# Where the softmax, the splits of x and the token sums stand around the end of the attention stage of a fused attention and two-layer MoE kernel

## What is computed

```
out_up    = repeat(softmax_attention(mean of 4 positions of q, k, v), 4)    # 144 x 144 per head
out_local = softmax_attention(q, k, v, only where |i - j| < 4)
x  = (out_up + out_local) as [2304, 512]
xn = x / sqrt(mean(x * x over 512) + 1e-6) * rms_g
y  = (silu(xn @ w_gate) * (xn @ w_val)) @ w_out                             # 512 -> 1536 -> 512
r  = maximum(y @ w_in, 0);  out = (r * r) @ w_out2                          # 512 -> 2048 -> 512
```

## Time and profile before

| | us |
|---|---|
| timed executions | 944.83, 945.67, 957.65; median 945.67 |
| profiled execution, its own time | 942.91 |
| its span | 941.1 |
| mean granted clock of TensorE | 0.992 of full |
| TensorE busy | 916.4 (97%) |
| DVE, ScalarE, GpSimd busy | 644.5, 447.3, 595.9 |

### The profile page before, as it was taken

The page is one execution under the profiler, slowest core; times in us unless marked ns, Lnnn a source line. Parts: engine busy times, 40 slices in busy tenths (PEclk is TensorE's granted clock), DMA queues, the critical chain, the costliest instruction groups (busy, mean ns, idle before and its releaser), DMA issues.

```text
span 941.1 us, 17729 instructions
## 1 busy us (share of the span) xinstructions
PE 916.4 (97%) x6056; PEld 829.9 (88%) x6056; DVE 644.5 (68%) x964; ACT 447.3 (48%) x1147; POOL 595.9 (63%) x627
## 2 busy tenths in 40 slices
PE   7999989999999999999999999999999999999998
PEld 6777778999989999989999988898989898989896
DVE  7999956789885778875555796667864466744443
ACT  4788965444565444465444465242533233423221
POOL 3688778787888778877777764556564445544420
PEclk9998989999999999999999999999999999999999
DMA  9965012222111111111111221212030101030101
GB/s 256 261 172 165 21 57 79 69 68 68 46 46 46 45 47 46 45 46 46 46 45 46 91 68 46 90 45 68 23 112 24 46 23 46 23 112 23 46 1 67
DMA packets 57673, 63.94 MB, mean 68 GB/s; under 512 B 5616, under 2 KB 50544, under 8 KB 57200
## 3 DMA queue, kind: packets, MB, share of 16 engines
q1 hardware_dynamic: 56000, 61.63, 22.3%
q10 hardware_dynamic: 1584, 1.18, 0.4%
HBM read 58.07 MB, written 4.72 MB: 67 GB/s over the span
## 4 chain that ended last, share of the span: by engine, by line
PE 78%; DVE 3%; issue 1%; ACT 1%; POOL 0%; DMA 0%; ACTq 0%; DVEq 0%
PE bank L1460 43%; PE bank L1515 21%; PE bank L1490 14%; DVE xs L1100 1%; DVE prod L1173 0%; ACT xs L753 0%; DVE vt L1167 0%; ACT wst L717 0%; PE bank L1470 0%; POOL wst L595 0%; DVE wst L1107 0%; DMA out_dram<-xT 0%; DVE gt L1167 0%; DVE wo L1212 0%; ACT xT L836 0%
## 5 line engine op out<-in xcount | busy, mean ns | idle before, releaser
L1460 PE MATMUL bank<-xs,wst 128*128 128x384 f32 x2520 | 503.2, 339 | 4.8 <-DVE vt L1167 2.1
L1460 PEld LDWEIGHTS bank<-xs,wst 128*128 128x128 f32 x2520 | 441.0, 188 | 28.9 <-issue 7.5
L595 POOL TENSOR_TENSOR wst<-wraw,wst 128x256 fp32r<-128x256 f32 x240 | 233.6, 991 | 126.1 <-ACT wst L717 124.4
L1515 PE MATMUL bank<-wo,gs 128*128 128x512 f32 x864 | 218.4, 393 | 1.4 <-ACT xT L836 0.8
L1490 PE MATMUL bank<-hb,wo 128*128 128x512 f32 x864 | 189.0, 336 | 1.3 <-DVE hb L1185 1.3
L1515 PEld LDWEIGHTS bank<-wo,gs 128*128 128x128 f32 x864 | 160.4, 188 | 29.8 <-DVE gs L1206 1.1
L1490 PEld LDWEIGHTS bank<-hb,wo 128*128 128x128 f32 x864 | 146.0, 188 | 9.9 <-issue 1.6
L1167 DVE TENSOR_TENSOR vt<-u,bank 128x384 f32<-128x384 f32 x120 | 66.2, 552 | 123.8 <-PE bank L1460 123.7
L717 ACT CAST wst<-wraw 128x256 fp32r<-128x256 f32 x360 | 123.4, 406 | 4.9 <-DMA wraw<-w_dram 2.7
L578 POOL TENSOR_TENSOR wraw<-wraw,stage 128x256 f32<-128x256 f32 x60 | 50.1, 835 | 105.9 <-DMA wraw<-w_dram 105.7
L797 ACT ACTIVATE sig<-gt 128x384 f32<-128x384 f32 x72 | 37.8, 526 | 121.4 <-DVE gt L1167 120.3
(11 more groups left out here) (110 smaller groups left out, 1034.2 us busy)
## 6 DMA issues: line engine op xcount, KB each, us to landing
wraw<-w_dram SPq DMA_DIRECT2D x180, 128.0 KB, 2.3
stage<-w_dram SPq DMA_DIRECT2D x60, 128.0 KB, 2.2
woraw<-w_dram SPq DMA_DIRECT2D x28, 256.0 KB, 3.0
vquad<-v_dram SPq DMA_DIRECT2D x16, 288.0 KB
out_dram<-xT SPq DMA_DIRECT2D x18, 256.0 KB, 3.0
vwin<-v_dram SPq DMA_DIRECT2D x28, 140.0 KB
kp<-k_dram SPq DMA_DIRECT2D x3, 1152.0 KB, 9.8
qs<-q_dram SPq DMA_DIRECT2D x3, 1152.0 KB, 15.3
```

The costliest lines, as they stand in the source:

```text
L595: nc.gpsimd.tensor_tensor(b[:, 1, :], w_source(w, p), b[:, 0, :].bitcast(fp32), ALU.subtract).then_inc(wlp_done, 1)
L1460: last = mm(XY[s % 2][:, 0:HC], wst[:, u % 2, p, pw, 128 * k:128 * k + 128], xs[:, p, px, k, :], start=(p not in CONTINUES and i == 0 and ...
L1515: last = mm(ACC[t][:, :], gs[:, v % 2, m, px, 128 * t:128 * t + 128], wo[:, 2 * j + m, pw, :], start=(j == 0 and n < 18 and i == 0), stop= ...
```

## The change

- The six token sums leave unit 37 and stand in pairs in units 36, 37 and 38. The 12 root steps of DVE start in unit 39 instead of 38.
- Attention's loop: ScalarE casts parts 0 and 1 of x in units 49 and 50; before, all seven stood in units 48 to 51. DVE subtracts part 0 in unit 50 only; before, parts 0 to 3 in units 49 to 51. GpSimd's two combinations of x go from units 49 and 50 to 48 and 51.
- Tail: ScalarE's other five casts and DVE's subtractions 1 to 4 stand between the attention's last steps, with the sums of unit 51 before most of them. GpSimd normalises unit 51 before its first subtraction of x. TensorE makes each group of unit 0's products one attention unit later.

```
-SUMS_AT = 37
-ROOT_AT = (38, 38, 39, 39, 39, 39, 40, 40, 40, 40, 41, 41)
+SUMS_AT = (36, 36, 37, 37, 38, 38)
+ROOT_AT = (39, 39, 39, 39, 40, 40, 40, 40, 41, 41, 41, 41)
...
-COMBINE_X_AT = (48, 49, 49, 50)
-X_HIGH_AT = (48, 49, 49, 50, 50, 51, 51)
-X_LOW_AT = (49, 50, 50, 51)
+COMBINE_X_AT = (48, 49, 48, 51)
+X_HIGH_AT = (49, 50)
+X_LOW_AT = (50,)
...
 # GpSimd, tail
+            normalise(G_ALL - 1)
             x_low(5)
-            normalise(G_ALL - 1)
             x_low(6)
...
 # ScalarE, tail
             keep_output(G_ALL - 6)
             take_turned(G_ALL - 4)
-            first_copy(0)
+            x_high(0, 2)
             keep_output(G_ALL - 5)
             take_turned(G_ALL - 3)
+            x_high(0, 3)
+            first_copy(0)
             keep_output(G_ALL - 4)
-            copy_11(0)
+            x_high(0, 4)
             take_turned(G_ALL - 2)
             keep_output(G_ALL - 3)
+            x_high(0, 5)
+            copy_11(0)
             take_turned(G_ALL - 1)
+            x_high(0, 6)
+            keep_output(G_ALL - 2)
             sigmoid(0, 0)
-            keep_output(G_ALL - 2)
             keep_output(G_ALL - 1)
...
 # DVE, tail
+            x_low(0, 1)
+            sums(G_ALL - 1)
+            x_low(0, 2)
+            x_low(0, 3)
             x_low(0, 4)
             add(0, 1)
-            sums(G_ALL - 1)
             for p in range(3, NP):
                 add(0, p)
...
 # TensorE
-            def token_sums():
-                pe.wait_ge(ss_add, 3)
-                pe.wait_ge(exp_done, FOUR_BANKS)
-                for t in range(TT):
-                    last = mm(SS[:, t:t + 1], ssq[:, 128 * t:128 * t + 128], ones[:, 0:1], start=True, stop=True,
-                              skip_group_check=True)
-                last.then_inc(ss_mm, 1)
+            def token_sums(t):
+                if t == 0:
+                    pe.wait_ge(ss_add, 3)
+                    pe.wait_ge(exp_done, FOUR_BANKS)
+                last = mm(SS[:, t:t + 1], ssq[:, 128 * t:128 * t + 128], ones[:, 0:1], start=True, stop=True,
+                          skip_group_check=True)
+                if t == TT - 1:
+                    last.then_inc(ss_mm, 1)
...
-                if g == SUMS_AT:
-                    token_sums()
+                for t in range(TT):
+                    if SUMS_AT[t] == g:
+                        token_sums(t)
...
             transposes(G_ALL - 4)
             values(G_ALL - 5)
-            product(0, 0)
             transposes(G_ALL - 3)
             values(G_ALL - 4)
+            product(0, 0)
+            transposes(G_ALL - 2)
+            values(G_ALL - 3)
             product(0, 1)
             product(0, 2)
-            transposes(G_ALL - 2)
-            values(G_ALL - 3)
+            transposes(G_ALL - 1)
+            values(G_ALL - 2)
             product(0, 3)
             product(0, 4)
-            transposes(G_ALL - 1)
-            values(G_ALL - 2)
+            values(G_ALL - 1)
             product(0, 5)
             product(0, 6)
-            values(G_ALL - 1)
```

More of the change, by code:

```diff
@@ L773, in _ @@
                     squares(0, SQUARES_AT.index(g))
-                for p in range(NP):
+                for p in range(len(X_HIGH_AT)):
                     if X_HIGH_AT[p] == g:
```

## The result

The changed kernel is slower, by little: a median of 956.55 us (12 executions, 946.21 to 960.32) against 946.23 for the kernel before in the same session (12 executions, one of them of 5052.8 us, which no mean below has in it); ratio 1.0075, 95% interval 1.0049 to 1.0102. A second session gave 955.45 against 949.89, ratio 1.0041 (1.0005 to 1.0076). The means from here on leave out the six executions that lay over 1.5% above the fastest of their kernel and count as slow. Over its two sessions the changed kernel's mean is 954.4 us (23 executions, 955.2 and 953.6); the kernel before has 948.0 in the first session (11 executions) and 949.2 to 950.0 in four later ones of 29 to 35. The forecast was 944.9, 0.8 us faster, in 940.8 to 949.5.

What follows compares the result with a forecast made beforehand. TensorE, busy 97%, was taken as the bound up to product (2,1), with GpSimd's chain binding after (0,3). Terms 0.25 + 1.5 + 1.5 - 2.5 = 0.75, say 0.8 us off the 945.67 median, gave 944.9 us, range 940.8 to 949.5.

Steps and rivals of the forecast that it cites:

- Part 1: Token sums spread over units 36 to 38: slow stretch there goes, 1.5 us gained, bounds 0 and 2.8.
- moved: Rival: grown wait at the second spread lowers the clock near 106 us; 1.9 us won, 943.8; chance 0.15.
- the likeliest case: Whole kernel: the parts sum to about 0.8 us won, median 944.9 us; chance 0.35.
- I take it that the clock stays up: Spread-out sums, units 36 to 38: full clock is kept, worth 2.8 us on TensorE, at most 3.4.
- Part 2: ScalarE's order, units 48 to 51: fewer casts, so transpose 48's second half starts at 121.1 instead of 122.55 us.
- DVE's work up to there is unchanged: Up to the maxima for unit 49's exponent (115.22 us): unit 48's removed cast brings nothing at first.
- Part 3: Softmax's tail up to product (0,3): 1.5 us won at full clock, 2.5 us lost to half clock.
- 1.5 us are won at full clock: Tail: product (0,3) ends at 131.8 us instead of 133.3.
- Half clock follows again: After the tail's waits, values 47 to about product (0,1) run at half clock, costing 2.5 us.
- Part 4: Product (0,3) to (2,1): GpSimd's chain bounds it, 15.5 us, shortened by only 0.25; TensorE's gain is lost waiting.
- The slower rival: New slow stretch in unit 2 after waits ahead of (2,0) and (2,1): 2.6 us slower, 948.2; chance 0.25.

Runs made afterwards that it cites:

- e1: Kernel before with only the change's token sums and root steps: 953.9 us mean, ratio 1.0051.
- before_again: Second profile of the kernel before, unchanged: 949.98 us.
- e8: Kernel before with only the change's token sums and root steps, and the second spread in unit 47 instead of 46: 950.1 us mean, ratio 0.9987.
- e11: As e10, but GpSimd's combination of x back in unit 49 instead of 48: 945.2 us mean, ratio 0.9941.
- e10: Changed kernel with token sums over 64 columns and unread matmuls filling waits at the second spread, values 46, transposes 48 and 49: 947.8 us mean, ratio 0.9986.
- e7: Changed kernel with unread matmuls filling waits at the second spread, values 46, transposes 48 and 49; one-column sums: 950.5 us mean, ratio 0.9995.
- e9: Kernel before with token sums over 64 columns and unread matmuls at the second spread, values 46 and transposes 48: 947.1 us mean, ratio 0.9969.
- e14: The kernel of e9 timed once more: 945.4 us mean, ratio 0.9959 against the kernel before.
- after_again: Changed kernel once more, unchanged, for a second profile: 953.6 us mean, ratio 1.0041 against the kernel before.
- e4: Kernel before with only the second spread one unit earlier, 45 in place of 46: 954.1 us mean, ratio 1.0037.
- after: First session and profile of the changed kernel: median 956.55 us, ratio 1.0075 against the kernel before.
- e2: The change without its token sums and root steps, which stay as in the kernel before: 952.3 us mean, ratio 1.0026.

## Why the prediction was wrong

**Part 1.** "That is the gain of part 1: 1.5 us." The size of the wait was right: 1.92 us in place of 0.92, where I had 2.2. What failed is its price. The forecast's own sum has it as the part of the gain that doesn't get through, with no clock in it; only the rival "moved" (this very wait) lowers the clock there, with a chance of 0.15. And that rival prices it as a gain on the forecast: 1.5 us late at units 48 to 51, against 2.5 us saved later. (Its sum should read 0.75 - 1.5 + 2.5 = 1.75 us won, not 1.9.) I priced slow stretches by the two in my trace, 6.7 us each. In three profiles with a wait of 1.9 us (both of the changed kernel, and e1) the stretch lasted 27 to 31 us, over all the attention that was left. At half clock the small matmuls of the attention held TensorE busy nearly throughout, so the waits of the earlier trace rows vanished, and the work took up to twice as long. From the second spread to product (2,1) it is 47.0 us in e1, whose tail is the old one, against 41.8 in before_again: 5.2 us lost where the rival had 1.0 won. In the changed kernel it is 8.6 us. The place was right, and half clock after the wait too; its length and so its price were wrong, and the likeliest case left it out.

The gain itself isn't there either. "I take it that the clock stays up" held in the changed kernel's profiles and e1's and failed in six others; in the mean the spread-out sums are worth nothing (e8), because a slow stretch began at sums of one column in six of nine profiles with three units of them, and in four of five with one. At sums of 64 columns it did in none of four.

**Part 2.** "DVE's work up to there is unchanged" was the second failing step. It was unchanged in its list, but not in its neighbour: I had GpSimd's combination in my account as work and didn't check what it would meet. With the combination moved back (e11), ScalarE's copies of transposes 46 and 47 stand 7.6 and 10.4 us behind the start of qk 48, as my 117.60 and 120.45 less 110.0 have them, and product (0,3)'s load is issued 21.9 us behind it (137.02 - 115.12), where my sum at full clock has the product's end at 131.8 - 110.0 = 21.8. In e10 and e7 the load is at 23.1, so the collision cost 1.2 us. The prediction quoted the rule for it, the shared port pair of the Trainium skill (SBUF — State Buffer, SBUF: two separate sides), and used it on the chain behind (0,3) only. The trace agrees with the rule: both instructions have two SBUF inputs, and the later one came out longer by about what it had to wait (1.2 us longer, 1.35 from its start to the end of GpSimd's).

**Part 3.** In the changed kernel's profile, which is at half clock there, the sums of unit 51 can't be judged; in e11 they come 12.5 us behind the start of qk 48, where I had 12.7. "1.5 us are won at full clock" set a new tail at full clock against an old one that was partly slow. The old order at full clock has that load at 22.5 us (e9, e14), so the new one wins 0.6 at like clock, with the collision taken out. "Half clock follows again" held for the unfilled waits: at the softmax's end every profile without fills in the tail has slow time, 7 to 14 us of it, unless the long stretch already covers it.

**Part 4** held in most profiles, though not in the one shown first. From the load behind product (0,3) to product (2,1) it is 15.3 us in the kernel before (133.57 to 148.86). With the new tail it is 14.8 to 15.0 in eight profiles of ten, after_again among them: 0.3 to 0.5 shorter, where I expected 0.25. TensorE's wait on GpSimd there is then 0.6 us as before, and the rest of its idle time lies ahead of it (0.74 and 0.89 us on DVE in after_again). In the changed kernel's first profile and in e10 it is 15.5: GpSimd's four additions take 6.2 to 6.3 us instead of 5.5, two of the four 1.9 to 2.0 us long instead of one, and TensorE waits 1.8 us, where I expected about 2. In either case what TensorE won was lost there, as said.

**The slower rival** (a slow stretch in unit 2, chance 0.25) named the right sign at the wrong place, which is luck and not insight: no profile has a slow stretch there, after waits of 0.66 and 1.84 us among dense products. The Trainium skill's warning on short idles between groups of matmuls (TensorE: Matmul & The Clock Gate, A second HAM failure mode: psum-queue depth-cycling) fits the attention, where the wait at the spread shows it (full clock up to 114.8 us and half from 114.9 in the changed kernel, full throughout in e10 with the wait filled), and not the products.

**The base.** One profile and three times were too few for a kernel whose executions spread over 13 us. The forecast of 944.9 lies 3 to 5 us below the means of the kernel before (948.0 to 950.0). That isn't what put the result outside the range: in its own session the kernel before had a median of 946.23, 0.6 above the 945.67 that I took, and the changed one 956.55. With the base 4.3 us higher the range would end at 953.8, still under both medians of the changed kernel.

## What to carry to other kernels

Take a part of work off TensorE's path and it arrives earlier at its next wait; where it works in small matmuls, that wait can cost several times its length, by the clock (here 1 us more of waiting, 5 us lost in e1's profile). Look at what it arrives at, and if nothing useful fits, fill the wait with matmuls nobody reads, or give thin ones more columns where that costs next to nothing. And when a GpSimd instruction is moved, look at DVE's list in its new place, not only at its own queue.

## What was not expected of the hardware

- A stretch at half clock had no one length in the attention: 3 us (e4 after the spread, before_again at the sums), 10 us (e8) and 29 us or more (after) were seen, with TensorE busy all through. What ends one within the attention stays open. The three long ones ended among unit 0's products.
- An idle of 0.9 to 4.9 us in which TensorE waits for nothing that the profile shows, near 20, 30 or 55 us, is in every profile, and slow stretches of 3 to 21 us begin near it in all but the first profile of the kernel before. It is there in both kernels, and differs from execution to execution. It wasn't treated here.
- Waits among dense products left the clock alone: 0.66 and 1.84 us around product (2,0) in the changed kernel. So did one wait of 1.57 us in the attention (e2), while half clock followed the three of 1.9 us there.
